# A sparse attention and expert kernel: its opening blocks joined, its first routing round counted tile by tile, and its early loads moved

## What is computed

```python
# attention: 4 batches x 8 heads, 768 positions, 64 per head
keep = (pos_k < n_global) | ((0 <= rel) & (rel < n_local))     # 8 and 96
dist = where(is_global & ~is_local, n_local, abs(rel))
scores = q @ k.T / 8 - slope[head] * dist, or -1e9 where not keep
x = softmax(scores) @ v                                        # 3072 x 512
# a dense layer
x = silu(x @ w_in) @ w_out                                     # 2048 inside
# eight experts, at most 384 tokens each
logits = x @ w_gate        # pairs (token, expert) taken by falling logit
out[tokens of e] = relu(x @ w1[e]) @ w2[e]                     # 1024 inside
```

## Time and profile before

| | us |
|---|---|
| median of 3 runs | 1107.69 (1106.57 to 1108.35) |
| the profiled execution | 1110.33 |
| its span | 1108.7 |
| TensorE busy | 1052.6 (95%) |
| VectorE busy | 639.4 (58%) |
| ScalarE busy | 455.2 (41%) |
| GpSimd busy | 422.2 (38%) |

### The profile page before, as it was taken

How to read it: one execution, slowest core, us unless ns; L and a number is a source line. 1 busy time by engine, 2 the same in 40 slices (tenths; PEclk the granted TensorE clock), 3 DMA queues, 4 the chain that set the end, 5 groups by cost and what they waited for, 6 DMA issues and landing times. The chain is left out here.

```text
span 1108.7 us, 20102 instructions
## 1 busy us (share of the span) xinstructions
PE 1052.6 (95%) x7416; PEld 899.7 (81%) x7416; DVE 639.4 (58%) x2268; ACT 455.2 (41%) x1167; POOL 422.2 (38%) x473
## 2 busy tenths in 40 slices
PE   7899999999999999999999999937999999999998
PEld 5677888888888888888888889836778777878987
DVE  5854747565656656565656553356767767766210
ACT  3765444444444444444444433202234334333442
POOL 1253222222222222222222222216377565586873
PEclk9999999999999999999999999958999999999999
DMA  6663212111212121111121000005045233433420
GB/s 186 207 208 130 74 54 73 48 71 55 73 54 73 54 73 41 64 54 71 54 74 54 30 10 20 1 20 180 27 183 181 106 133 122 177 111 132 191 105 29
DMA packets 19140, 99.90 MB, mean 90 GB/s; under 512 B 2800, under 2 KB 2800, under 8 KB 16848
## 3 DMA queue, kind: packets, MB, share of 16 engines
q0 software_dynamic: 9824, 58.99, 15.2%
q1 hardware_dynamic: 9216, 39.61, 10.7%
HBM read 86.00 MB, written 12.85 MB: 89 GB/s over the span
## 5 line engine op out<-in xcount | busy, mean ns | idle before, releaser
L382 POOL TENSOR_TENSOR g_low<-g,g_high 128x256 fp32r<-128x256 f32 x192 | 152.3, 794 | 468.4 <-ACT g_high L586 468.2
L480 PE MATMUL up_ps<-x_high,w_high 128*128 128x256 f32 x768 | 227.7, 296 | 4.5 <-DVE g L733 4.5
L480 PE MATMUL up_ps<-x_low,w_high 128*128 128x256 f32 x768 | 216.4, 282 | 0.0
L480 PE MATMUL up_ps<-x_high,w_low 128*128 128x256 f32 x768 | 216.2, 282 | 0.0
L733 DVE SCALAR_TENSOR_TENSOR g<-g,up_ps 128x256 f32<-128x256 f32 x192 | 80.3, 418 | 206.8 <-ACT g L579 206.8
L586 ACT ACTIVATE g_high<-g 128x256 fp32r<-128x256 f32 x192 | 80.2, 418 | 231.0 <-PE down_ps L493 124.6
L480 PEld LDWEIGHTS up_ps<-x_high,w_high 128*128 128x128 f32 x768 | 145.0, 189 | 15.6 <-issue 7.7
L493 PE MATMUL down_ps<-w_high,g_high 128*128 128x512 f32 x384 | 152.1, 396 | 0.0
L493 PE MATMUL down_ps<-w_high,g_low 128*128 128x512 f32 x384 | 151.7, 395 | 0.0
L493 PE MATMUL down_ps<-w_low,g_high 128*128 128x512 f32 x384 | 151.6, 395 | 0.0
L480 PEld LDWEIGHTS up_ps<-x_low,w_high 128*128 128x128 f32 x768 | 145.2, 189 | 2.8
(11 more groups left out here) (204 smaller groups left out, 1864.8 us busy)
## 6 DMA issues: line engine op xcount, KB each, us to landing
qk_t<-qk_rows SPq DMA_DIRECT2D x24, 720.0 KB, 4.4
v_w<-v_win SPq DMA_DIRECT2D x24, 464.0 KB
w_raw<-weights SPq DMA_DIRECT2D x16, 512.0 KB, 7.1
x_rest<-x_any POOLq DMA_DIRECT2D x24, 256.0 KB, 3.0
x_rows<-x POOLq DMA_DIRECT2D x12, 512.0 KB, 3.2
w_raw<-gate_rows SPq DMA_DIRECT2D x1, 2048.0 KB, 7.1
x_g<-x_rows,token_index POOLq DMA_INDIRECT x24, 3.6
out<-y,token_index POOLq DMA_INDIRECT x24, 2.7
```

The lines of the kernel that those rows point to most:

```text
L382: pool.tensor_tensor(g_low[:, u % 2, :], g[:, u % 2, :], g_high[:, u % 2, :].bitcast(F32), ALU.subtract)\
L480: last = nc.tensor.matmul(up_ps[:, u % 2, 0:GT * P], a[:, f, w], x[:, grp % 2, c, :], start=k == 0, stop=k == 3 * C - 1)
```

## The change

Four edits in one. (1) The three opening blocks become one: nothing meets between them, `beyond_made` is what the branch waits for, and the engines meet by a semaphore inside the slow attention alone, if it is taken. The bias tables are made in `prepare`, ahead of the branch, by a shorter formula; ScalarE makes heads 2 and 3; VectorE makes heads 4 to 7 behind shifts 0 and 1. There are 18 unread matmuls in place of 9, and a small exponential and a small reduction that nobody reads. (2) Pair 0's queries and keys of row 0 are asked for first, ahead of the wait for the limits; row 1's loads wait for the first shift; the values of row 2 go ahead of weights 2 and 3; first rows load their used part only. (3) From step 12 on the scaling goes ahead of `rest_x`, and the weights' split behind tanh, silu, high and low part of the step's first chunk. (4) In round 0 of the routing one tile is counted at a time, all counts fall in one place, and the subtraction goes; the clearing of `cmp` shrinks to one column and goes to the end of GpSimd's preparation.

```diff
-        self.rel, self.kpos, self.local, self.dist, self.keep, self.masked = (
-            scratch[:, (k + 2) * SPAN:(k + 3) * SPAN] for k in range(6))
+        self.rel, self.kpos, self.ahead, self.dist = (scratch[:, (k + 2) * SPAN:(k + 3) * SPAN] for k in range(4))
+        self.limits_i = sb("limits_i", [P, 2, 2], I32)
...
             sp.dma_start(limits_i[:, 0, :], n_global.partition_broadcast(P)).then_inc(limits_in, 16)
             sp.dma_start(limits_i[:, 1, :], n_local.partition_broadcast(P)).then_inc(limits_in, 16)
+            sp.dma_start(first.qk_t[:, 0, 0, 0:2 * P], qk_rows[0, :, 0, 0:2 * P]).then_inc(first.qk_first_in, 16)
             sp.wait_ge(limits_in, 32)
-            sp.dma_start(first.qk_t[:, 0, :, :], qk_rows[0, :, :, :]).then_inc(first.qk_in[0], 16)
-            sp.dma_start(first.v_w[:, 0, :, :, :, :], v_win[0, :, :, :, :, :]).then_inc(first.v_in[0], 16)
+            sp.dma_start(first.qk_t[:, 0, 1:, 0:2 * P], qk_rows[0, :, 1:, 0:2 * P]).then_inc(first.qk_in[0], 16)
+            sp.dma_start(first.v_w[0:P // 2, 0, :, :, :, :], v_win[0, 0:P // 2, :, :, :, :]).then_inc(first.v_in[0], 16)
...
-                      channel_multiplier=0).then_inc(first.offsets_made, 1)
+                      channel_multiplier=0).then_inc(offsets_made, 1)
+            pool.wait_ge(first.qk_first_in, 16)
             pool.dma_start(x_stand_in, some_rows).then_inc(first.stand_in, 16)
             pe.wait_ge(ident_made, 1)
-            for _ in range(9):
+            for _ in range(18):
                 nc.tensor.matmul(unread[:, 0:P], ident[:, :], ident[:, :], start=True, stop=True)
+
+        @block.scalar
+        def _(act):
+
+            act.wait_ge(ident_made, 1)
+            nc.scalar.activation(unused[:, 0, :], ident[:, 0:8], ACT.Exp)
...
+            rel, kpos, ahead, dist, local = first.rel, first.kpos, first.ahead, first.dist, first.local
+            dve.wait_ge(ident_made, 1)
+            v.tensor_tensor_reduce(out=unused[:, 1, :], in0=ident[:, 0:8], in1=ident[:, 8:16], scale=1.0, scalar=0.0,
+                                   op0=ALU.add, op1=ALU.min, accum_out=past[:, 0:1])
+            dve.wait_ge(offsets_made, 1)
+            v.tensor_copy(kpos, first.offsets[:, 1, :])
+            link(v.tensor_copy(rel, first.offsets[:, 0, :]))
+
+            link(v.tensor_scalar(ahead, rel, 0.0, float(1 << 20), ALU.is_lt, ALU.mult))
+            link(v.tensor_tensor(rel, rel, ahead, ALU.add))
             dve.wait_ge(limits_in, 32)
...
-            v.tensor_copy(beyond[:, :], past[:, 0:1])
+            v.tensor_copy(beyond[:, :], past[:, 0:1]).then_inc(first.beyond_made, 1)
+
+            link(v.tensor_scalar(dist, kpos, limits[:, 0:1], UNSEEN, ALU.is_ge, ALU.mult))
+            v.tensor_scalar(local, rel, limits[:, 1:2], None, ALU.is_lt)
+            link(v.tensor_scalar(dist, dist, limits[:, 1:2], None, ALU.max))
+            v.copy_predicated(dist, local, rel).then_inc(first.dist_made, 1)
+            dve.wait_ge(first.dist_made, 1)
+            for h in range(2):
+                last = v.tensor_scalar(first.bias8[:, h, :], dist, first.slopes8[h], None, ALU.mult)
+            last.then_inc(first.bias_ready, 1)
...
             def load_qk(row):
 
                 reached(sp, qk_done, (row - 1) * PAIRS)
-                sp.dma_start(qk_t[:, row % 2, :, :], qk_rows[row, :, :, :]).then_inc(qk_in[row % 2], 16)
+                used = P + keys_of(row)[1]
+                sp.dma_start(qk_t[:, row % 2, :, 0:used], qk_rows[row, :, :, 0:used]).then_inc(qk_in[row % 2], 16)
...
+                part, _ = keys_of(row)
+                sp.dma_start(v_w[0:part, row % 2, :, :, :, :], v_win[row, 0:part, :, :, :, :])\
+                    .then_inc(v_in[row % 2], 16)
...
+            sp.wait_ge(scores_ready, 2)
             load_qk(1)
             load_v(1)
             load_weights(0)
+            sp.wait_ge(bias_ready, H // 2 - 1)
+            sp.wait_ge(pair_bias_ready, 1)
+            load_weights(1)
             load_qk(2)
-            sp.wait_ge(bias_ready, H // 2)
-            for f in range(1, RAW):
+            load_v(2)
+            for f in range(2, RAW):
                 load_weights(f)
-            sp.dma_start(gate[:, :, :], gate_t).then_inc(gate_in, 16)
...
-                if row is not None and row + 2 < ROWS:
+                if row is not None and 0 < row < ROWS - 2:
                     load_v(row + 2)
...
+                if n == LEAD:
+                    sp.dma_start(gate[:, :, :], gate_t).then_inc(gate_in, 16)
...
-                for f in split_in(n):
-                    if not rest_on_vector(f):
+                rests = [f for f in split_in(n) if not rest_on_vector(f)]
+                if n < LEAD:
+                    for f in rests:
                         rest_w(f)
                 for m in chunks_of(n):
                     if m % FC == 1 and 0 <= m // FC - 1 < G:
                         store_x2(m // FC - 1)
                     if chunk_there(m + AHEAD):
                         rest_g(m + AHEAD)
+                    if n >= LEAD and m % 2 == 0:
+                        for f in rests:
+                            rest_w(f)
...
+                if u == 0:
+                    pe.wait_ge(first.qk_first_in, 16)
+                elif u == 1 or (pair == 0 and row > 0):
                     pe.wait_ge(qk_in[row % 2], 16 * (row // 2 + 1))
...
-                    unread_products({0: 10, 1: 3}.get(n, 0))
+                    unread_products({0: 6, 1: 3}.get(n, 0))
...
+            act.wait_ge(first.dist_made, 1)
+            for h in (2, 3):
+                last = nc.scalar.activation(bias8[:, h, :], first.dist, ACT.Copy, scale=first.slopes8[h])
+            last.then_inc(pair_bias_ready, 1)
...
-                for f in split_in(n):
-                    if n != LEAD - 1:
+
+                if n < LEAD - 1:
+                    for f in split_in(n):
                         round_w(f)
                 for m in chunks_of(n):
                     if n == LEAD - 1:
                         round_w(split_in(n)[m % 2])
                     if chunk_there(m + AHEAD):
                         half_tanh(m + AHEAD)
+                    if n >= LEAD and m % 2 == 0:
+                        for f in split_in(n)[:1]:
+                            round_w(f)
                     if m == -2:
                         keep_turned(LEAD - 2)
                     if chunk_there(m + AHEAD):
                         round_g(m + AHEAD)
+                    if n >= LEAD and m % 2 == 0:
+                        for f in split_in(n)[1:]:
+                            round_w(f)
                     if m == -1:
                         keep_turned(LEAD - 1)
...
-            def distances():
-                link(v.tensor_scalar(local, rel, limits[:, 1:2], None, ALU.is_lt))
-                link(v.scalar_tensor_tensor(local, rel, 0.0, local, ALU.is_ge, ALU.mult))
-                v.scalar_tensor_tensor(dist, rel, limits[:, 1:2], local, ALU.subtract, ALU.mult)
-                link(v.scalar_tensor_tensor(keep, kpos, limits[:, 0:1], local, ALU.is_lt, ALU.max))
-                v.tensor_scalar(masked, keep, 1.0, -MASKED, ALU.subtract, ALU.mult)
-                link(v.scalar_tensor_tensor(dist, dist, limits[:, 1:2], keep, ALU.add, ALU.mult))
-
             def bias(pair):
                 for h in range(2 * pair, 2 * pair + 2):
-                    slope8 = -8.0 * 2.0 ** (-8.0 * (h + 1) / H)
-                    last = v.scalar_tensor_tensor(bias8[:, h, :], dist, slope8, masked, ALU.mult, ALU.add)
+                    last = v.tensor_scalar(bias8[:, h, :], first.dist, first.slopes8[h], None, ALU.mult)
                 last.then_inc(bias_ready, 1)
 
...
-                if row == 0:
-                    dve.wait_ge(bias_ready, pair + 1)
+                if row == 0 and pair == 1:
+                    dve.wait_ge(pair_bias_ready, 1)
+                elif row == 0:
+                    dve.wait_ge(bias_ready, max(pair, 1))
...
-            distances()
             for n in range(STEPS):
-                if n < PAIRS:
-                    bias(n)
                 if n < LEAD:
                     shift(n)
+                if n + 2 < PAIRS:
+                    bias(n + 2)
...
                 if 1 <= n < LEAD:
                     scale_probs(n - 1)
+                for u in scored_in(n):
+                    scale_probs(u)
                 if row is not None:
                     rest_x(row)
                 if n == LEAD - 1:
                     scale_probs(n)
-                for u in scored_in(n):
-                    scale_probs(u)
-
-                for f in split_in(n - 1 if n < LEAD - 1 else n):
-                    if rest_on_vector(f):
+
+                rests = [f for f in split_in(n - 1 if n < LEAD - 1 else n) if rest_on_vector(f)]
+                if n < LEAD:
+                    for f in rests:
                         rest_w(f)
                 for m in chunks_of(n):
                     if chunk_there(m + AHEAD):
```

(60 more changed lines are left out.)

152 lines of the change are left out of this document (82 added, 70 removed).

## The result

The changed kernel takes 1103.28 us (median of 20 runs, 1097.46 to 1109.27) against 1109.01 (median of 20, 1105.04 to 1111.76). The ratio is 0.9948, 95% interval 0.993 to 0.9966: 5.7 us faster by the medians, not 12.4. The spread has grown from 7 to 12 us. Every run has its mean granted clock of TensorE beside it, and time goes with clock: 0.984 for the run of 1097.46, 0.969 for the one of 1109.27.

The account below looks back on a forecast made before the run. Bound by TensorE from 300 to 600 us, with gaps at the start, splitting and routing; 4.9 lead-in + 5.7 splitting + 1.8 routing = 12.4 us, from the median 1107.69 to 1095.2 us (chance 0.54), range 1091 to 1101.

Parts of the forecast that it names:

- the clock of the lead-in: Start up to first up product: warm-up matmuls end at 10.1 us at half clock, earlier if it rises; no loss priced.
- First shift: Opening: bias, branch and TensorE each ready by about 10.7 us for 15.82, a gain of 5.1 us, bounds 4 and 6.5.
- My rival on it: Opening: the 3.03 us idle comes twice or late, first shift at 12.5; gain 10.6, time 1097.1 us; chance 0.12.
- Units 0 to 3: Lead-in, shift 0 to shift 4: 8.07 us become 7.5, 0.5 us gained.
- Loads: Lead-in: row 1's keys and keys 2 are asked for later, 0.7 us lost, bounds 0 and 5.
- The right rival: Lead-in loads: every transfer keeps its 10.1 us, about 4.9 us lost; gain 7.5, time 1100.2 us; chance 0.14.
- Lead-in as a whole: Start to first up product: 5.1 + 0.5 - 0.7 = 4.9 us gained.
- Splitting: Weight-splitting steps from 12 on: waits for silu and the half clock behind them go; gain 5.7 us, bounds 3 and 6.5.
- Routing: Routing's first round: subtractions go (1.3 us), full clearing goes (0.5 us), single-tile matmuls come out even; 1.8 us gained.
- The rival that one-tile matmuls cost a pair's slot: Routing: 24 matmuls each take a pair's time; gain only 7.9 to 8.5, time 1099.5 us; chance 0.08.
- my first bound: Routing: a pair costs 0.053 us, mostly weights, so a 31-column load costs half and the level comes out even.
- The slower rival: Weight loads: buffer reuse waits longer, a loop past 14.1 us; at 6 us over, 18 us lost, 1113 us; chance 0.04.

Follow-up runs that it names:

- part 3 alone: The kernel before with only the new order in the splitting steps; 1102.43 us against 1108.79 for the kernel before beside it, ratio 0.9946.
- part 4 alone: The kernel before with only the routing's first round counted tile by tile; 1105.61 us against 1110.48 for the kernel before beside it, ratio 0.997.

## Why the prediction was wrong

- **The step that failed: the clock of the lead-in.** I wrote that no row would be under 1.00 from the first up product to the routing, and for the opening asked only whether TensorE's warm-up ended in time. I never priced the line that cuts the unread products from 10 to 6. I went through what the change adds and moves, and passed over a removal. With 6, TensorE was idle for 2.14 us, and half clock for 23.5 us followed. First up product 36 to 38 forecast; 45.3 in both profiles, 39.3 and 41.0 with 14 products, 38.0 with the keys earlier as well. That the removal cost the time is shown by putting products back (0.9948 and 0.9941 with 6, 0.9911 and 0.9912 with 14). What made the half clock last so long stays open: 2.02 us of idle with 10 products had only 3.4 us of it. Four more us went in the experts' products, at half clock from 772 to 786; no term of mine was there, and their cause is open too.
- **First shift:** 10.7 forecast, 12.20 measured; 3.6 us won of 5.1. I had the 3.03 us of idle gone or moved; it came back as 3.58 between bias and first shift, which I had named as a sign of being wrong. My rival on it named this wait, put the shift at 12.5, and priced it at 1.8 us, close to the 1.5 it took; but the small reduction, which it charged with 3 us at the start, took 0.17.
- **Units 0 to 3:** 7.5 forecast from shift 0 to shift 4; 7.41 with 14 products (11.98 to 19.39). Right, where the clock is full; 10.66 at half clock, and 8.8 to 9.0 in three profiles with 14 products in which half clock came for 3.4 us at 15 us.
- **Loads:** row 1's keys were in time in every profile. I had 0.7 us lost; from unit 4's shift to the first up product the kernel with 14 products took 19.88 us against 18.09, so 1.8 lost, and 18.33 with the keys earlier. The right rival in the wrong row: it was row 2's keys behind two weights, 12 us from issue (16.90) to scores (28.93), near the 10.1 of the earlier trace rows.
- **Lead-in as a whole:** 4.9 forecast; 2.7 and 1.0 in the two profiles with 14 products, 4.0 with the keys earlier, minus 3.4 in the changed kernel's own.
- **Splitting:** 5.7 forecast, 6.4 measured; the 0.5 kept back for collisions was not needed.
- **Routing:** 1.8 forecast, 2.0 measured: 1.4 from the seven levels, in every profile. The 0.7 ahead of them is less sure: kernels with the same code there differ by up to 1.3 us from profile to profile. The rival that one-tile matmuls cost a pair's slot is out: 0.033 us each at half clock (0.80 / 24), and 24 of them take what 12 pairs take, my first bound. There I had also put 60 cycles at 1.2 GHz on the Trainium skill's account; its table ("TensorE: Matmul & The Clock Gate", "Back-to-back issue gap") is for 2.4 GHz and names a floor of 25 ns, which the 33 ns respect.
- **Sum:** 12.4 forecast (from the median that is 1095.3, not 1095.2); 9.9 by the ratio with 14 products, 12.8 with the keys earlier as well. That the last is so near is partly luck: it is another program, and its lead-in is 0.9 short while splitting and routing are 0.9 over. The best of the changed kernel's 20 runs (1097.46) was inside my range. The missing products took 3 to 4 us by the ratios, and 6 by the medians of the chip on which both ran.
- **The slower rival** (weight loads) showed nowhere: first up product to last down product took 671.5 to 673.2 us in all 13 profiles with the new order, and 676.4 to 678.1 in the five with the old one.

## What to carry to other kernels

Treat matmuls that nobody reads as work with a purpose: when a change shortens or moves the wait that they fill, look in the timeline where TensorE now stands still, and try the fill at several counts again. Ask of a lead-in what it becomes at half clock: filling the gap was worth 3 to 4 us in the tightened kernel and nothing that could be told in the one before, whose lead-in hung on VectorE. If the runs spread more than before, read the mean clock of each run before the median, and judge an edit by the length of its own stretch.

## What the runs showed of the hardware that was not expected

- The same program falls to half clock or doesn't, from run to run: 22 of 33 runs with 6 unread products had a mean clock of 0.979 or less, and 4 of 41 with 14 or more (all with the new splitting order).
- Like gaps had unlike sequels. In the kernel before TensorE idled 1.9 us up to 16.4 us and half clock lasted some 3 us; in the changed one 2.14 us of idle were followed by 23.5 us of it, with TensorE busy for 22.57. So it was in its second profile (2.06) and with the old order (2.09); 2.02 us with 10 products had 3.4, and 3.29 us with the keys earlier 6.8. In the three long cases the warm-up matmuls had ended at 8.7 to 8.8 us, in the two others at 7.3 and 7.7; whether that has a part was not tested, and what ends such a stretch stayed open.
- In the experts' products the length of a wait went with the clock. TensorE's first wait for VectorE there, in a search of the routing (L1361 in the changed kernel), lasted 1.15 to 1.46 us in six profiles: one (the kernel before) had 3.4 us of half clock behind it, four had 10 to 14 us, one had none. In the twelve others it lasted 0.50 to 1.02 us, and no half clock followed. The four are the changed kernel twice, with 10 products, and with 6 and the keys earlier. What sets the length of this wait is not shown. The changed kernel, then the second profile with 14 products:

```profile
771.51 0.18 PE L1361 MATMUL search_ps<-steps_col,reached_any 128*128 128x1 bf16 x1 [1.39 <-DVE reached_any L1606]
...
766.16 0.18 PE L1361 MATMUL search_ps<-steps_col,reached_any 128*128 128x1 bf16 x1 [0.50 <-DVE reached_any L1606]
```

- VectorE idles 1.4 to 3.7 us for instructions near its first shift, and how long differs between kernels that have the same instructions there (3.03 before, 2.62 with part 3 alone, 1.44 with part 4 alone, which edits a stretch 700 us later). There is one profile of each, so edit and chance can't be told apart; two profiles of the same kernel differed by 0.05 and 0.31 us.
